# Attention with a threshold and two mixing layers: the order of SyncE's transfers in an attention pair, and filler matmuls at the start

## The chip, the core and the metric

One core of a Trainium2 chip runs the whole kernel. Its engines are TensorE (PE in the rows, with PEld for its weight loads), VectorE (DVE), ScalarE (ACT), GpSimd (POOL) and SyncE (SP), whose instructions here only issue transfers to the core's DMA engines. The metric is the time of one execution in microseconds (us), the median of several.

## The reference

Eight batches of eight heads, 576 positions, head size 64. Attention keeps only the scores within tau of their row's maximum:

```python
scores = scale * np.matmul(q, k.transpose(0, 1, 3, 2))          # (8, 8, 576, 576)
thresh = np.max(scores, axis=-1, keepdims=True) - tau
scores = np.where(scores >= thresh, scores, -1000000000.0)
attn = np.exp(scores - np.max(scores, axis=-1, keepdims=True))
attn = attn / (np.sum(attn, axis=-1, keepdims=True) + 1e-09)
x = np.matmul(attn, v)                                          # then (8, 576, 512)
```

Two mixing layers follow on x. The first mixes each position with the one before it, multiplies by w_k (512 to 1024), squares the positive part, multiplies by w_v, and gates the result with a sigmoid of a product with w_r. The second gates x @ w_val with the sigmoid of a causal convolution over five positions, and multiplies by w_out.

## The kernel before

The attention stage comes first, then the mixing stage, which starts when attention has ended. Attention works on 32 **pairs** of heads; in pair c both heads share the 128 partitions. Its scores are made in nine tiles, scores0 to scores8, of 128 rows by 576 columns each, in three PSUM slots.

Each engine has a written-out order of steps for one turn of the loop, `run(it, c)`; a step marked `-` in a plan belongs to the pair before. In turn c:

- **TensorE** follows `PE_PLAN`: probs5 of the pair before, then scores1, k0, kq0 (transposes of the next pair's k and of the remainders), scores0, pv0 of the pair before (the product with v), q0, and so on. `scores1` is the first product that needs the stacked q and k of its pair.
- **VectorE** takes a tile's maximum (L651), later its mask with the row sum (L656), and once a pair, between mask8 of the pair before and mask1, the reciprocal of all row sums (L662).
- **ScalarE** takes the exponential (L586) and copies every transposed tile out of PSUM (L568, L572).
- **GpSimd** has one queue of work in each turn. With `with_w` (24 turns, c - 3 counts them) it begins with one block of the mixing weights, which it splits into a high and a low part:

```python
def run(it, c, with_w=False):
    if with_w:
        split_w(it, c - 3)          # waits for w_stage (L414, L416)
    if c > 0:
        sums(it, c - 1)             # row_sum + 1e-9 (L421); the reciprocal waits for it
    if c < PAIRS - 1:
        split_k(it, c + 1, c)       # k_hi, k_lo of the next pair (L405, L408)
        if c == 0:
            wait(q_stacked[0], 32)
        split_q(it, c + 1, c)       # q_hi, q_lo of the next pair (L394, L396)
    if c > 0:
        normalize(it, c - 1)        # x_out = x_raw * recip_rows (L429, L432)
```

- **SyncE** issues, in program order and waiting where a transfer's source isn't ready: q and k of pair c + 2 (`load_q`, `load_k`, six transfers), the reciprocals of pair c - 1 to DRAM (`send_recip`, two), the halves of k_lo and k_hi of pair c + 1 that change partitions (`stack_k`, four), the same for q (`stack_q`, L257 and L258, waits for q_lo), the reciprocals of pair c - 1 back as rows spread over partitions (`fetch_rows`, L320, two transfers), v of pair c + 1 (`load_v`, three), a block of weights into the single buffer `w_stage` (`load_w`, L300, one) and x of pair c - 1 to DRAM (`store_x`, L305, waits for x_out).

At the very start TensorE has nothing to do while the first q and k arrive, are transposed and split. `keep_busy(n)` issues n products of the identity with itself into a score slot, whose result nobody reads; each shows as two matmuls in the trace. `FIRST_PREPARE` is the steps k0, kq0, q0; it runs for pair 0 and then for pair 1, ahead of the first scores.

Of the kernel before, what the change touches and what calls it, by code (L numbers as in the profile page):

```python
# [21 lines left out]
def steps(text):  # L22

    return [(w.rstrip("-")[:-1], int(w.rstrip("-")[-1]), w.endswith("-")) for w in text.split()]
# [16 lines left out]
FIRST_PREPARE = steps("k0 kq0 q0")  # L41
# [40 lines left out]
def attention(nc, q, k, v, tau, small_loads, x_first, weights, x_scratch, recip_scratch, w_hi, w_lo):  # L82

    B, H, S, D = q.shape
    PAIRS = B * H // 2
# [9 lines left out]
    with ExitStack() as ctx:  # L95
# [78 lines left out]
        def count(it, c, per_pair, local):  # L174
            return it * (2 * per_pair) + (c * per_pair + local)
# [33 lines left out]
        def turns(it, n):  # L209
            return it * (2 * PER_PAIR) + n  # L210
# [33 lines left out]
        def load_q(eng, it, c):  # L244
            load_qk(eng, 0, "q", it, c, q_loaded)
# [7 lines left out]
        def stack_q(eng, it, c):  # L253

            par = c % 2
            eng.wait_ge(q_steps, count(it, c, 3, 3))
            eng.dma_start(q_all[REM:P, par, 0:QW].bitcast(F32), q_lo[0:REM, :].bitcast(F32)).then_inc(q_stacked[c % 2], 16)  # L257
            eng.dma_start(q_all[0:REM, par, H1:].bitcast(F32), q_lo[REM:P, :].bitcast(F32)).then_inc(q_stacked[c % 2], 16)  # L258
# [10 lines left out]
        with nc.Block() as block:  # L269

            @block.sync
            def _(sp):
# [18 lines left out]
                def load_w(it, c, w, at):  # L291


                    n = c - 2
                    sp.wait_ge(w_split, count(it, n, 2, 2))
                    if w.shape[1] == UNIT:
                        rows, col = it * (2 * P) + (n - at) * P, 0
                    else:
                        rows, col = it * P - at // 2 * P, n * UNIT
                    sp.dma_start(w_stage[:], w[bass.ds(rows, P), col:col + UNIT]).then_inc(w_loaded, 16)  # L300
# [14 lines left out]
                def fetch_rows(it, c):  # L315

                    rows = recip_scratch[c % 2]
                    sp.wait_ge(recip_stored, count(it, c, 32, 32))
                    for h in range(2):
                        sp.dma_start(recip_rows[D * h:D * (h + 1), :],  # L320
                                     rows[h].partition_broadcast(D)).then_inc(rows_loaded, 16)

                def run(it, c, *weight):
                    if c <= PAIRS - 3:

                        sp.wait_ge(aux_full, turns(it, prepared(c - 1)))
                        load_q(sp, it, c + 2)
                        load_k(sp, it, c + 2)
                    if c > 0:
                        send_recip(it, c - 1)  # L330
                    if c < PAIRS - 1:
                        stack_k(it, c + 1)
                        stack_q(sp, it, c + 1)
                    if c > 0:
                        fetch_rows(it, c - 1)
                    if c < PAIRS - 1:
                        if c > 0:
                            sp.wait_ge(aux_full, turns(it, number_of(c - 1, "pv", 1) + 1))
                        load_v(sp, it, c + 1)
                    if weight:  # L340
                        load_w(it, c, *weight)
                    if c > 0:
                        store_x(it, c - 1)

# [117 lines left out]
            def _(pe):  # L462
# [89 lines left out]
                def keep_busy(n):  # L552


                    for _ in range(n):
                        nc.tensor.matmul(score_ps[2][:, 0, 0:P], ident[:], ident[:], start=True, stop=True)
# [1 line left out]
                keep_busy(9)  # L558
                run(FIRST_PREPARE, 0, -1)
                keep_busy(3)  # L560
                run(FIRST_PREPARE, 0, 0)
                keep_busy(3)
                walk(run, pe, PE_PLAN)

            @block.scalar
# [652 lines left out]
```

## Time and profile before

| | |
|---|---|
| median of 3 runs | 1316.13 us (1315.88 to 1316.9) |
| profiled execution | 1318.56 us, of which the span of its instructions is 1316.7 us |
| PE busy | 1282.7 us, 97% of the span |
| DVE busy | 886.7 us, 67% |
| ACT busy | 842.7 us, 64% |
| POOL busy | 334.5 us, 25% |
| mean share of the clock granted to TensorE | 0.99 |

The times of the runs are of whole executions; the trace covers the span of one of them. A busy share is a mean over the attention stage (roughly the first 585 us) and the mixing stage, which have different limits. PE's busy time counts the whole passage of overlapping matmuls through the array, so a busy PE isn't necessarily one without room.

### The profile page before, as it was taken

To read this page: it belongs to the slowest core of one execution; us is meant where nothing else is said; L and a number is where in the kernel's file an instruction comes from. 1 tells how busy PE (TensorE), PEld (TensorE's weight loads), DVE (VectorE), ACT (ScalarE), POOL (GpSimd) and SP (SyncE) were. 2 spreads that over 40 slices of the span, in tenths; PEclk is the share of its full clock that TensorE was granted. 3 is DMA by queue.
4 is the path that set the end of the run, shared out by engine and by line. 5 is a ranking of instruction groups with operands and counts; after the bars stand their busy time and mean duration, and the time that the engine had idled before them with its cause. 6 is when DMAs were issued, how large, how long until landed. Compare 5 with 4: busy or idle time off the path is not lost.

```text
span 1316.7 us, 29536 instructions
## 1 busy us (share of the span) xinstructions
PE 1282.7 (97%) x9358; PEld 1134.5 (86%) x9358; DVE 886.7 (67%) x1969; ACT 842.7 (64%) x2023; POOL 334.5 (25%) x385
## 2 busy tenths in 40 slices
PE   7999999999999999979999999999999999999998
PEld 6778777777777777759999999999989999999997
DVE  4777777777777777758666665657655766566644
ACT  4888888888888888866544453445445544544432
POOL 2466555666665554512000000000000000000000
PEclk7999999999999999999999999999999999999999
DMA  6455656665656655421001101110110011001000
GB/s 148 109 148 151 158 152 158 155 155 151 149 148 161 161 146 144 120 80 53 9 27 36 35 9 37 35 35 1 35 44 18 19 35 35 17 27 35 17 9 33
DMA packets 137821, 105.19 MB, mean 80 GB/s; under 512 B 92416, under 2 KB 109056, under 8 KB 137728
## 3 DMA queue, kind: packets, MB, share of 16 engines
q1 hardware_dynamic: 136224, 103.41, 29.4%
q8 instruction: 49, 0.80, 0.3%
q10 hardware_dynamic: 1504, 0.62, 0.2%
q14 instruction: 44, 0.36, 0.1%
HBM read 54.56 MB, written 19.02 MB: 56 GB/s over the span
## 4 chain that ended last, share of the span: by engine, by line
PE 54%; ACT 0%; DVE 0%; issue 0%; DVEq 0%
PE kv_ps L894 16%; PE kv_ps L975 15%; PE vr_ps L894 15%; PE y_ps L959 8%; ACT mixed L1007 0%; DVE x L1146 0%; ACT xm_hi L1015 0%; ACT y L1024 0%; DVE mixed L1087 0%; DVE square L1104 0%; DVE g_lo L1119 0%; DVE x_lo L1151 0%; DVE xm_lo L1093 0%; DVE gated L1114 0%; ACT g_hi L1055 0%
## 5 line engine op out<-in xcount | busy, mean ns | idle before, releaser
L656 DVE SCALAR_TENSOR_TENSOR probs<-score_ps,threshold,probs 128x576 f32<-128x576 f32 x288 | 227.9, 808 | 44.3 <-ACT probs L586 44.2
L651 DVE TENSOR_REDUCE neg_max<-score_ps 128x1 f32<-128x576 f32 x288 | 211.8, 753 | 53.9 <-PE score_ps L505 53.9
L586 ACT ACTIVATE probs<-score_ps,neg_max 128x576 f32<-128x576 f32 x288 | 213.5, 741 | 0.0
L505 PE MATMUL score_ps<-k_lo,q_all 128*128 128x288 f32 x640 | 195.7, 335 | 8.1 <-DVE probs L656 6.7
L568 ACT ACTIVATE probsT<-aux_ps 128x512 f32<-128x512 f32 x288 | 165.1, 600 | 38.2 <-PE aux_ps L466 33.9
L466 PE MATMUL aux_ps<-ident,probs 128*128 128x128 f32 x1280 | 185.0, 276 | 0.1
L505 PE MATMUL score_ps<-k_hi,q_all 128*128 128x288 f32 x640 | 173.8, 299 | 0.0
L466 PEld LDWEIGHTS aux_ps<-ident,probs 128*128 128x128 f32 x1280 | 150.7, 141 | 17.1 <-ACT probsT L568 15.2
L894 PE MATMUL kv_ps<-xm_hi,w_lo 128*128 128x288 f32 x512 | 152.0, 297 | 10.3 <-DVE xm_lo L1093 7.3
L894 PE MATMUL kv_ps<-xm_hi,w_hi 128*128 128x288 f32 x512 | 152.1, 297 | 0.0
L894 PE MATMUL kv_ps<-xm_lo,w_hi 128*128 128x288 f32 x512 | 151.9, 297 | 0.0
L975 PE MATMUL kv_ps<-kk_hi,w_hi 128*128 128x288 f32 x512 | 151.1, 295 | 0.0
L975 PE MATMUL kv_ps<-kk_lo,w_hi 128*128 128x288 f32 x512 | 150.9, 295 | 0.0
L975 PE MATMUL kv_ps<-kk_hi,w_lo 128*128 128x288 f32 x512 | 150.2, 293 | 0.0
L1159 DVE SCALAR_TENSOR_TENSOR gate<-x,taps,gate 128x288 f32<-128x288 f32 x256 | 132.1, 516 | 18.8 <-ACT gate L1044 15.3
L546 PE MATMUL aux_ps<-probsT,v_nat 128*64 128x320 f32 (+1 forms) x1024 | 138.3, 412 | 2.9 <-ACT probsT L568 1.2
L884 POOL MEMSET x_in<- 128x4 f32 x7 | 0.7, 106 | 539.2 <-DVE mixed L1087 539.2
L505 PEld LDWEIGHTS score_ps<-k_lo,q_all 128*128 128x128 f32 x640 | 119.2, 192 | 15.4 <-DVE probs L656 13.2
L505 PEld LDWEIGHTS score_ps<-k_hi,q_all 128*128 128x128 f32 x640 | 119.9, 193 | 0.0
L546 PEld LDWEIGHTS aux_ps<-probsT,v_nat 128*64 128x64 f32 x1024 | 68.8, 136 | 52.7 <-issue 6.4
L1044 ACT ACTIVATE gate<-x,taps 128x288 f32<-128x288 f32 x64 | 34.1, 533 | 115.4 <-DVE x L1146 115.4
L894 PEld LDWEIGHTS kv_ps<-xm_hi,w_lo 128*128 128x128 f32 x512 | 97.2, 190 | 11.5 <-DVE xm_lo L1093 7.9
(93 smaller groups left out, 2953.4 us busy)
## 6 DMA issues: line engine op xcount, KB each, us to landing
q_all<-q_lo SPq DMA_DIRECT2D x62, 160.0 KB, 2.6
recip_rows<-recip_scratch SPq DMA_DIRECT2D x64, 144.0 KB, 3.2
x_scratch<-x_out SPq DMA_DIRECT2D x32, 288.0 KB, 2.1
out<-y SPq DMA_DIRECT2D x36, 256.0 KB, 2.0
v_nat<-in_v SPq DMA_DIRECT2D x32, 256.0 KB, 2.9
qk_nat<-in_q SPq DMA_DIRECT2D x63, 128.0 KB, 2.6
qk_nat<-in_k SPq DMA_DIRECT2D x63, 128.0 KB, 2.6
k_hi<-k_hi SPq DMA_DIRECT2D x32, 160.0 KB, 2.6
```

The source lines that it names most:

```text
L466: return nc.tensor.transpose(out, in_, ident[:])
L505: last = nc.tensor.matmul(ps[:, half, 0:HALF], query(h, i, par), kk[:, par, at:at + HALF], start=(n == 0), stop=(n == len(terms) - 1))
L546: last = nc.tensor.matmul(bank[D * h:D * (h + 1), 0:cols.stop - cols.start], v_nat[rows, cc % 2, h * FULL + t if t < FULL else MIX, :], m, ...
L568: return nc.scalar.activation(out, in_, ACT.Copy)
L586: nc.scalar.activation(tile_halves(i), scored(i), ACT.Exp, bias=neg_max[:, i:i + 1], scale=1.0).then_inc(exp_done, 1)
L651: nc.vector.tensor_reduce(neg_max[:, i:i + 1], scored(i), mybir.AxisListType.XY, ALU.max, negate=True).then_inc(max_ready, 1)
L656: nc.vector.scalar_tensor_tensor(tile_halves(i), scored(i), threshold[:, i:i + 1], tile_halves(i), ALU.is_ge, ALU.mult, accum_out=row_sum[ ...
L894: last = nc.tensor.matmul(ps, w, m, start=(n == 0), stop=(n == 3 * len(terms) - 1))
L959: last = nc.tensor.matmul(y_ps[i % 2][:], g[:, ch, col:col + P], w[:, ch, :], start=(n == 0), stop=(n == 3 * C - 1))
L975: last = nc.tensor.matmul(kv_ps[u][:, 0:HT], w, m[:, j, :], start=(n == 0), stop=(n == 3 * CF - 1))
L1044: nc.scalar.activation(gate[:, i, :], x2[:, i, 0:HT], ACT.Copy, scale=taps[:, 0, i:i + 1]).then_inc(conv_begun, 1)
L1159: nc.vector.scalar_tensor_tensor(gate[:, u, :], x2[:, u, t:t + HT], taps[:, t, u:u + 1], gate[:, u, :], ALU.mult, ALU.add).then_inc(conv_s ...
```

## The change

SyncE's order in a turn is changed in two places. `fetch_rows` now stands ahead of `stack_q`, and `load_w` ahead of `load_v` and of the wait that guards `load_v`. The transfers themselves, their sizes and what they wait for are the same. On TensorE the fillers at the start change: fifteen now stand between kq0 and q0 of pair 1, and seven where three stood ahead of the first scores.

```diff
                     if c < PAIRS - 1:
                         stack_k(it, c + 1)
-                        stack_q(sp, it, c + 1)
                     if c > 0:
                         fetch_rows(it, c - 1)
+                    if c < PAIRS - 1:
+                        stack_q(sp, it, c + 1)
+                    if weight:
+                        load_w(it, c, *weight)
                     if c < PAIRS - 1:
                         if c > 0:
                             sp.wait_ge(aux_full, turns(it, number_of(c - 1, "pv", 1) + 1))
                         load_v(sp, it, c + 1)
-                    if weight:
-                        load_w(it, c, *weight)
                     if c > 0:
                         store_x(it, c - 1)
...
                 keep_busy(3)
-                run(FIRST_PREPARE, 0, 0)
-                keep_busy(3)
+                run(FIRST_PREPARE[:-1], 0, 0)
+                keep_busy(15)
+                run(FIRST_PREPARE[-1:], 0, 0)
+                keep_busy(7)
                 walk(run, pe, PE_PLAN)
```

This is SyncE's queue in a turn of the loop with weights, before the change; the names are destination and source of a transfer, and the rows without DMA compute addresses and semaphore values.

```order
L279 DMA k_hi<-k_hi 64x640
L256 ISA
L257 DMA q_all<-q_lo 64x640
L258 DMA q_all<-q_lo 64x640
L318 ISA
L320 DMA recip_rows<-recip_scratch 64x576 x2
L338 REGISTER_ALU
L219 ISA
L219 DMA v_nat<-in_v 128x2x256
...
L300 ISA
L300 DMA w_stage<-in_moe_w_k 128x512
```

And this is the same place after the change.

```order
L279 DMA k_hi<-k_hi 64x640
L318 ISA
L320 DMA recip_rows<-recip_scratch 64x576 x2
L256 ISA
L257 DMA q_all<-q_lo 64x640
L258 DMA q_all<-q_lo 64x640
L295 REGISTER_ALU
L300 ISA
L300 DMA w_stage<-in_moe_w_k 128x512
L341 REGISTER_ALU
L219 ISA
L219 DMA v_nat<-in_v 128x2x256
```

The two row fetches have moved ahead of the two q copies, and the weight block ahead of the three transfers of v. Turns without weights show the same move without the L300 rows.

TensorE's queue at the start, before the change, from the fillers between the preparations of pair 0 and pair 1 (`ident,qk_nat` x4 is k0 the first time and q0 the second, `ident,rem_nat` is kq0):

```order
L556 MATMUL score_ps<-ident 128x128 x3
L466 MATMUL aux_ps<-ident,qk_nat 128x128 x4
L466 MATMUL aux_ps<-ident,rem_nat 128x128
L466 MATMUL aux_ps<-ident,qk_nat 128x128 x4
L556 MATMUL score_ps<-ident 128x128 x3
L505 MATMUL score_ps<-k_lo,q_all 128x288
```

After the change:

```order
L557 MATMUL score_ps<-ident 128x128 x3
L467 MATMUL aux_ps<-ident,qk_nat 128x128 x4
L467 MATMUL aux_ps<-ident,rem_nat 128x128
L557 MATMUL score_ps<-ident 128x128 x15
L467 MATMUL aux_ps<-ident,qk_nat 128x128 x4
L557 MATMUL score_ps<-ident 128x128 x7
L506 MATMUL score_ps<-k_lo,q_all 128x288
```

Fifteen fillers now precede q0 of pair 1, and the run of fillers ahead of the first score product has grown from three to seven.

## Rows read from the trace of the kernel before

**Rows 1.** Windows, with and without weights: us, busy us (instructions) by engine.

```profile
53.60:476.10 422.50, 417.16 (x3225) 322.86 (x3222) 320.16 (x673) 371.42 (x866) 259.31 (x289) 1.00 0.60 154
...
492.40:561.30 68.90, 68.55 (x535) 53.15 (x535) 53.69 (x112) 60.89 (x143) 35.70 (x41) 1.00 0.51 133
```

**Rows 2.** Waits, 53.7 to 476 us: total us, times, longest.

```profile
POOL x_out L429 <- DMA recip_rows<-recip_scratch: 103.4, 19, 7.3
DVE recip L662 <- POOL row_sum L421: 36.6, 24, 2.4
...
PEld score_ps L505 <- DVE probs L656: 8.3, 19, 1.1
```

**Rows 3.** Waits, 476 to 561 us.

```profile
POOL row_sum L421 <- DVE probs L656: 8.8, 4, 2.5
```

**Rows 4.** Timeline of DVE: start, us, instruction, idle before and releaser.

```profile
53.64 0.21 DVE L662 RECIPROCAL recip<-row_sum 128x9 f32<-128x9 f32 x1 [0.44 <-POOL row_sum L421]
...
492.51 0.21 DVE L662 RECIPROCAL recip<-row_sum 128x9 f32<-128x9 f32 x1 [0.44 <-POOL row_sum L421]
...
561.38 0.21 DVE L662 RECIPROCAL recip<-row_sum 128x9 f32<-128x9 f32 x1 [0.45 <-POOL row_sum L421]
```

**Rows 5.** Timeline of POOL, one period of a pair with weights.

```profile
265.82 0.25 POOL L421 TENSOR_SCALAR row_sum<-row_sum 128x9 f32<-128x9 f32 x1
...
271.83 1.55 POOL L396 TENSOR_TENSOR q_lo<-q_raw,q_all 128x640 fp32r<-128x640 f32 x1
...
278.61 1.30 POOL L429 TENSOR_TENSOR x_out<-x_raw,recip_rows 128x512 f32<-128x512 f32 x1 [5.24 <-DMA recip_rows<-recip_scratch]
...
281.10 0.61 POOL L414 CAST w_hi<-w_stage 128x512 f32 x1 [0.92 <-DMA w_stage<-in_moe_w_v]
...
283.31 0.25 POOL L421 TENSOR_SCALAR row_sum<-row_sum 128x9 f32<-128x9 f32 x1
```

**Rows 6.** Timeline of SP's queue, the same period: start, us of issuing.

```profile
272.42 0.60 SPq L279 DMA_DIRECT2D k_hi<-k_hi  x1
...
273.40 0.46 SPq L257 DMA_DIRECT2D q_all<-q_lo  x1
...
274.62 1.15 SPq L320 DMA_DIRECT2D recip_rows<-recip_scratch  x2
...
278.13 0.36 SPq L300 DMA_DIRECT2D w_stage<-in_moe_w_v  x1
```

**Rows 7.** Landing times: the second q copy (L258).

```profile
DMA to landing us min/median/max: 2.6/2.7/4.0
```

**Rows 8.** Landing times: the row fetches (L320).

```profile
DMA to landing us min/median/max: 2.8/3.2/3.9
```

**Rows 9.** Timeline of SP's queue, a pair without weights.

```profile
516.63 0.60 SPq L279 DMA_DIRECT2D k_hi<-k_hi  x1
```

**Rows 10.** Timeline of PE, scores1 of the pair after it.

```profile
522.70 0.40 PE L505 MATMUL score_ps<-k_lo,q_all 128*128 128x288 f32 x1
```

**Rows 11.** Timeline of PE at the start: start, us, instruction, idle before.

```profile
7.96 0.83 PE L556 MATMUL score_ps<-ident 128*128 128x128 f32 x6
...
12.53 0.66 PE L466 MATMUL aux_ps<-ident,qk_nat 128*128 128x128 f32 x4 [3.19 <-ACT k_raw L568]
...
15.11 0.61 PE L505 MATMUL score_ps<-k_lo,q_all 128*128 128x288 f32 x1 [0.99 <-DMA q_all<-q_lo]
```

**Rows 12.** Windows around the clock's changes; PEclk stands after POOL.

```profile
13.40:13.50 0.10, 0.10 (x4) 0.10 (x3) 0.00 (x0) 0.10 (x1) 0.10 (x1) 0.72 1.01 149
...
30.50:31.00 0.50, 0.50 (x6) 0.50 (x5) 0.43 (x1) 0.37 (x2) 0.00 (x0) 0.99 0.00 0
```

**Rows 13.** Timeline of DVE at the start: the first maximum.

```profile
16.48 0.76 DVE L651 TENSOR_REDUCE neg_max<-score_ps 128x1 f32<-128x576 f32 x1 [5.34 <-PE score_ps L505]
```

**Rows 14.** Timeline, a score group and its maximum at the full clock.

```profile
270.16 0.38 PE L505 MATMUL score_ps<-k_lo,q_all 128*128 128x288 f32 x1
...
270.97 0.76 DVE L651 TENSOR_REDUCE neg_max<-score_ps 128x1 f32<-128x576 f32 x1 [0.49 <-PE score_ps L505]
```

## The prediction

> **What bounds the kernel now.** The change acts on the attention stage, so I read that stage alone, first as windows. Over the pairs with weights TensorE counts as busy for 417.16 of 422.50 us, over those without for 68.55 of 68.90; DVE and ACT have room in both [rows 1]. That looks like a stage bound by TensorE whatever SyncE does. But busy time counts overlapping passages, so I went on to how long a pair takes. The reciprocal comes once a pair. From 53.64 to 492.51 us there are 25 periods (the 24 with weights and the one that follows them), 438.87 us, 17.55 each; from 492.51 to 561.38 four without weights, 68.87 us, 17.22 each [rows 4]. The same products therefore take 0.33 us longer per pair when GpSimd also has a weight block to split, and this difference is what the change can reach.
>
> The waits name the place. With weights the reciprocal waits for GpSimd's row_sum 24 times, 36.6 us together, or 1.5 us each, where the hand-over alone costs 0.44 when GpSimd is in time [rows 2, 4]. TensorE's score weights wait for a mask 19 times, 8.3 us [rows 2]; that is the late reciprocal passed on, for mask1 stands behind it. Without weights it is the other way round: row_sum waits 2.2 us for VectorE (8.8 us in four) [rows 3].
>
> Why is GpSimd late? I followed one period back. row_sum starts at 265.82; the work behind it, the splits of k and q, ends with q_lo, which starts at 271.83 and takes 1.55, so 273.38 [rows 5]. At 273.40 SyncE issues the q copies, at 274.62 the row fetches, then v, and at 278.13 the weight block [rows 6]. GpSimd gets the rows at 278.61 and the weights at 281.10, and the next row_sum comes at 283.31 [rows 5]. This is a closed loop: 7.56 (row_sum to the end of q_lo) + 0.02 (the queue answers) + 1.22 (q copies) + 3.51 (row fetches and v) + 2.97 (the weights' flight) + 2.21 (split) = 17.49 us, the whole distance from 265.82 to 283.31. With weights the bound is thus a ring over GpSimd, SyncE's queue and one transfer, slightly longer than the 17.22 that the rest of the stage needs.
>
> **The change, part by part.** *Row fetches ahead of the q copies.* The fourth k copy is issued from 272.42 to 273.02 [rows 6]. Before, the queue then stood until q_lo was ready, at 273.40; now the fetches go at about 273.05, 1.57 us sooner, and rows that came at 278.61 come near 277.0. x_out and its small second part fill the time from 278.61 to about 280.2 now (1.6 us, its first part 1.30), so GpSimd would be free at 278.6. *Weights ahead of v.* Fetches to 274.2, q copies to 275.4, weight block issued at about 275.5 instead of 278.13. With the same flight of 2.97 it lands at 278.5, as GpSimd becomes free. Then 2.21 us of splitting puts row_sum at 280.8 instead of 283.31, 2.5 us sooner. It was 1.5 - 0.44 = 1.1 us late on average, so it will be in time with about 1.4 to spare, even in the worst turn (2.4 - 0.44 = 2.0 us late [rows 2]). The ring shrinks to about 15.0 us and stops binding. Next comes whatever gives the pairs without weights their 17.22. I take that value: (438.87 - 25 x 17.22) = 438.87 - 430.5 = **8.4 us gained**. Bounds: 0, if weights slow the stage in another way, and 9 or so, since nothing in rows 4 shows a pair faster than 17.2 for a reason that would stay.
>
> *v later.* Its three transfers slip by roughly 0.6 us in a turn with weights (one weight issue of 0.36 and its addresses), and are used a pair later; I cost this at nothing, covered by nearly a whole period. Without that cover it would be 0.6 us a pair.
>
> *The q copies later.* This is the price of the exchange. In a pair without weights the fourth k copy ends at 516.63 + 0.60 = 517.23 [rows 9]. Two fetches (1.15) and the first q copy (about 0.55) now stand ahead of the second q copy, with the gaps it is issued at about 519.2. With its median flight of 2.7 [rows 7] it lands at 521.9, and scores1 of the next pair begins at 522.70 [rows 10]: 0.8 us of room. Flight may grow behind 288 KB of fetches. The fetches, the nearest transfers that now fly behind others, take 3.2 [rows 8]; at 3.2 there is still 0.3. I cost it at nothing, with the bounds 0 and 0.5 us a pair (flight 4.0, the longest seen [rows 7]).
>
> The Trainium skill speaks to this ("DMA: Bandwidth & Descriptors", section "Queues, rings and completion order"): on each DMA engine the descriptors of one issuing queue are consumed in ring order. By that rule the q copies can't overtake the fetches, and every byte of these stands before them; the sum by the rule alone has the room of 0.8 us less whatever the fetches' data take, which brings the slower rival below nearer. The row of the second q copy, 2.7 us behind four k copies and a first q copy, shows that standing behind others cost little so far.
>
> *The fillers.* TensorE stood idle for 3.19 us ahead of q0 of pair 1, and the granted clock then fell to half inside the window at 13.40 and came back only inside 30.50 to 31.00 [rows 11, 12]. Six filler matmuls took 0.83 us at the full clock [rows 11], at a spacing of about 0.12 once the passage of the last is taken off. Fifteen fillers are 30 matmuls, 3.6 us, from about 9.2 to 12.8: they fill the idle time and push q0 from 12.53 to about 12.8. q0 isn't urgent, GpSimd comes to it after the k splits. Seven are 14 matmuls, 1.7 us, so TensorE is free at about 15.0, and the scores start at 15.11 as before, when the q copy has landed [rows 11]. If the fillers ran longer, 0.14 each, the scores would start 0.8 us late: that is the loss side. The gain: with the half clock the first maximum came 16.48 - 15.11 = 1.37 us after the first score product [rows 11, 13], at the full clock this takes 270.97 - 270.16 = 0.81 [rows 14]. That is 0.56 us at the first tile. In the idle-ridden stretch that follows VectorE sets the pace, and the clock may well fall again; if it stayed full to 30 us, I'd add two more such first tiles (1.1) and half of roughly 3 us of score and transpose work back to back: 2.8 in all. Between -0.8 and 2.8 I take **0.9**, near the term that I can name.
>
> **Sum.** 8.4 + 0.9 = 9.3 us. The profiled execution took 1318.56 us, 1316.7 of span and 1.86 around it; it would become 1309.3. It stands 2.43 above the median of the runs, so for the median 1316.13 - 9.3 = **1306.8 us**. One term without a sign: as the mixing stage begins, the clock's return depends on when the work falls, and may move the end by about 1 us either way (my estimate, from the 0.56 us that one tile at half clock costs).
>
> **The rivals.**
>
> *The q copies come too late.* Mechanism: scores1 waits for q_stacked at the head of every pair, some 30 pairs. It decides when the flight of the second q copy exceeds 522.70 - 519.2 = 3.5 us. At 4.0 each of 30 pairs loses 0.5 us, 15 us against 9.3 gained: 1321.8, slower. For it: the transfers are issued nearly as fast as they are served, and 4.0 has occurred. Against: 2.7 is the median and even the fetches take 3.2. Slower than before takes over 3.9 us; 5 in 100 for that, 5 more for a loss that eats only half the gain.
>
> *The weighted pairs keep part of their extra.* The ring is broken, but other waits, such as ScalarE's or the DMA engines' greater share with weights (0.60 against 0.51 [rows 1]), hold the period at about 17.4. Half of 8.4 is left, 1311.0. 14 in 100.
>
> *The change doesn't do it.* TensorE counts as busy 99% of the time both with and without weights [rows 1]; if that were its true load, earlier rows and weights would only give GpSimd idle time, and only the start would move: 1315.2. Against it stands the ring's sum, which equals the measured period. 7 in 100.
>
> *The clock holds through the first 30 us.* 8.4 + 2.8: 1304.9. 15 in 100. My forecast, 1306.8 within 2 us, keeps 54.
>
> **How the numbers follow.** The point is the forecast. The range of 8 in 10 reaches down past the case of the held clock with a share of the 1 us at the seam, to 1302.5, and up to cover the case of half the gain, 1312.5; outside are the unchanged case and the slow end of the late copies above, and something below. About 0.2%, 2.6 us, is what a measurement of this kernel tells from no change. Faster by more than that needs a time below 1313.5: 54 + 15 + 14 and half of the late copies, together 0.87; the same 0.08; slower 0.05.
>
> **What would show it right or wrong.** In the changed profile the reciprocal's idle time should be 0.44 in nearly all turns, row_sum should be released by VectorE's probs instead of following w_lo, and the reciprocal's period should be about 17.2 from the first turn to the last. The rows should reach GpSimd some 1.5 us sooner in a turn. Wrong would be a wait of PE's scores1 for the DMA q_all from q_lo, once a pair: then the exchange has made a new head of the ring. At the start PE's idle time ahead of q0 should be gone, the clock full past 13.40, and the first maximum at about 15.9 instead of 16.48.

## The result and the profile after

| | before | after |
|---|---|---|
| median | 1316.01 us (20 runs, 1313.73 to 1319.45 and one of 2775.76) | 1318.4 us (20 runs, 1316.31 to 1322.9) |
| ratio, 95% interval | | 1.0019 (1.0011 to 1.0027) |
| profiled execution | 1318.56 us, span 1316.7 | 1316.92 us, span 1315.1 |

The change makes the kernel 0.19% slower, 2.4 us by the medians, where I had forecast 9.3 us of gain. The one execution of 2775.76 us isn't part of the ratio. The two profiled executions stand the other way round: that of before is 2.5 us above its median, that of after 1.5 us below. A difference of 1.6 us between two profiles therefore doesn't carry the verdict. But the profiles show which stretch gained and which lost. From the head of the changed kernel's page, its span and the busy time of each engine:

```profile
span 1315.1 us, 29612 instructions
...
PE 1282.8 (98%) x9396; PEld 1136.1 (86%) x9396; DVE 891.0 (68%) x1969; ACT 839.9 (64%) x2023; POOL 334.5 (25%) x385
```

Busy times are nearly those of before. DVE has 4 us more with the same number of instructions, a first hint that some of them took longer; ACT has 3 us less. The timeline of DVE shows the reciprocals that answer to [rows 4], now with the last of the 32 as well:

```profile
53.56 0.21 DVE L665 RECIPROCAL recip<-row_sum 128x9 f32<-128x9 f32 x1 [0.45 <-POOL row_sum L422]
...
487.15 0.22 DVE L665 RECIPROCAL recip<-row_sum 128x9 f32<-128x9 f32 x1 [0.45 <-POOL row_sum L422]
...
556.59 0.21 DVE L665 RECIPROCAL recip<-row_sum 128x9 f32<-128x9 f32 x1 [0.45 <-POOL row_sum L422]
...
573.00 0.22 DVE L665 RECIPROCAL recip<-row_sum 128x9 f32<-128x9 f32 x1 [0.44 <-POOL row_sum L422]
```

and the last of the kernel before:

```profile
577.75 0.21 DVE L662 RECIPROCAL recip<-row_sum 128x9 f32<-128x9 f32 x1 [0.43 <-POOL row_sum L421]
```

The reciprocal waits 0.45 us, the bare hand-over, in every pair. From 53.56 to 487.15 there are 25 periods of 17.34 us where there were 17.55. From 487.15 to 556.59 there are four without weights, of 17.36, where there were 17.22. So the pairs with weights gained 0.21 us of the 0.33 that I expected, and those without lost 0.14 each. The first turn, from the first reciprocal (35.26 us) to the second, takes 18.30 us instead of 17.23: it gives back the 1.15 us that the start had won. The last reciprocal comes at 573.00 instead of 577.75 us, and yet the span is only 1.6 us shorter: from that row to the end it takes 742.1 us instead of 739.0. Something after the attention stage lost 3.1 us.

The timeline of POOL for one period with weights, to set against [rows 5]:

```profile
267.75 1.55 POOL L397 TENSOR_TENSOR q_lo<-q_raw,q_all 128x640 fp32r<-128x640 f32 x1
273.53 1.30 POOL L430 TENSOR_TENSOR x_out<-x_raw,recip_rows 128x512 f32<-128x512 f32 x1 [4.23 <-DMA recip_rows<-recip_scratch]
...
275.83 0.61 POOL L415 CAST w_hi<-w_stage 128x512 f32 x1 [0.73 <-DMA w_stage<-in_moe_w_v]
...
278.93 0.25 POOL L422 TENSOR_SCALAR row_sum<-row_sum 128x9 f32<-128x9 f32 x1 [0.98 <-DVE probs L659]
```

q_lo ends at 269.30. The rows come 4.23 us after that instead of 5.23, the weights 6.53 instead of 7.72, and the next row_sum is now released by VectorE, 0.98 us after GpSimd was ready for it. The old ring is open, as forecast. SP's queue around it, in the order of the change (start, us of issuing), to set against [rows 6]:

```profile
268.94 0.60 SPq L279 DMA_DIRECT2D k_hi<-k_hi  x1
269.66 1.16 SPq L320 DMA_DIRECT2D recip_rows<-recip_scratch  x2
270.94 0.51 SPq L257 DMA_DIRECT2D q_all<-q_lo  x1
271.50 0.60 SPq L258 DMA_DIRECT2D q_all<-q_lo  x1
272.39 0.34 SPq L300 DMA_DIRECT2D w_stage<-in_moe_w_v  x1
```

The second q copy is now issued at 271.50, 2.56 us after the issue of the last k copy began; before it went right behind the first q copy of 273.40, that is at 273.9, 1.5 us after the k copy of 272.42. The following lines belong to L258, the second q copy: who waited for it (us, times) and its flight, to set against [rows 7]:

```profile
  PE score_ps L506: 1.7, 6
...
DMA to landing us min/median/max: 2.7/3.5/3.9
```

Its flight has grown from 2.7 to 3.5 us, and PE's scores wait for it six times, 1.7 us together, the first of them at the start.

That count is too low: a wait for several semaphores is put down to only one of them. One pair as an example, the issue of its second q copy and the first weight load of its scores1:

```profile
392.67 0.59 SPq L258 DMA_DIRECT2D q_all<-q_lo  x1
...
396.73 0.19 PEld L506 LDWEIGHTS score_ps<-k_lo,q_all 128*128 128x128 f32 x1 [0.52 <-DVE probs L659]
```

This copy landed 3.85 us after its issue, at 396.52, and the weight load began 0.21 us later, after 0.52 us of idle time that is put down to DVE. I followed all 31 copies that SyncE issues. In the changed kernel TensorE's sequencer (the part that issues its instructions) already stood waiting when the copy landed in 29 of them; the weight load followed at a median of 0.21 us behind the landing, and the engine was idle ahead of it in 26, for 7.0 us together. In the kernel before this median was 1.8 us and the idle time 0.05. The length of a pair follows the landing: 17.21 us with a flight of 3.20 us, 17.29 with 3.55, 17.54 with 3.74, 17.70 with 3.85. So the q copy has become the new head of nearly every pair. At the start, timelines of PE and DVE, to set against [rows 11, 13]:

```profile
8.87 3.51 PE L557 MATMUL score_ps<-ident 128*128 128x128 f32 x30
...
12.65 1.73 PE L557 MATMUL score_ps<-ident 128*128 128x128 f32 x14
14.61 0.40 PE L506 MATMUL score_ps<-k_lo,q_all 128*128 128x288 f32 x1 [0.23 <-DMA q_all<-q_lo]
...
15.44 1.42 DVE L654 TENSOR_REDUCE neg_max<-score_ps 128x1 f32<-128x576 f32 x2 [4.70 <-PE score_ps L506]
```

On TensorE, the 30 filler matmuls took 3.51 us, the 14 took 1.73, close to the 3.6 and 1.7 of the forecast. The scores waited only 0.23 us, and the first maximum came 15.44 − 14.61 = 0.83 us after them.

**The seam between the stages.** This is the place that I had not followed. The mixing stage begins with VectorE and ScalarE preparing the first eight inputs (mixed, xm_hi, xm_lo), while GpSimd splits w_out, which SyncE has just begun to load. Two of VectorE's rows, GpSimd's first row of w_out and the window of 12 us from the first matmul of the stage (at 591.35), in the kernel before (a window's columns are those of [rows 1]: PE, PEld, DVE, ACT and POOL, then PEclk, DMA share and GB/s):

```profile
592.07 0.51 DVE L1087 SCALAR_TENSOR_TENSOR mixed<-x_in,mu,mixed 128x288 f32<-128x288 f32 x1
592.50 0.45 DVE L1093 TENSOR_TENSOR xm_lo<-mixed,xm_hi 128x288 fp32r<-128x288 f32 x1
...
593.10 1.12 POOL L876 CAST w_out_hi<-y 128x512 fp32r<-128x512 f32 x1 [4.00 <-DMA y<-in_moe_w_out]
...
591.35:603.35 12.00, 12.00 (x70) 11.76 (x71) 12.00 (x16) 6.78 (x18) 9.22 (x8) 0.76 0.34 109
```

And the same in the changed kernel, where the first matmul is at 586.74:

```profile
587.08 0.87 DVE L1096 TENSOR_TENSOR xm_lo<-mixed,xm_hi 128x288 fp32r<-128x288 f32 x1
587.87 1.52 DVE L1090 SCALAR_TENSOR_TENSOR mixed<-x_in,mu,mixed 128x288 f32<-128x288 f32 x1
...
586.93 0.71 POOL L879 CAST w_out_hi<-y 128x512 fp32r<-128x512 f32 x1 [2.44 <-DMA y<-in_moe_w_out]
...
586.74:598.74 12.00, 9.95 (x46) 8.91 (x47) 11.72 (x15) 5.96 (x16) 8.34 (x8) 0.61 0.20 57
```

Before, GpSimd's work on w_out's first block began 1.75 us after the first matmul; by then VectorE had got ahead of TensorE, 0.51 us a step. After the change it began 0.19 us after the first matmul, and VectorE's steps took 0.87 and 1.52 us from there on. TensorE starved, as its timeline in the changed kernel shows:

```profile
588.01 0.61 PE L897 MATMUL kv_ps<-xm_hi,w_lo 128*128 128x288 f32 x1 [0.18 <-DVE xm_lo L1096]
...
590.23 0.61 PE L897 MATMUL kv_ps<-xm_hi,w_lo 128*128 128x288 f32 x1 [1.14 <-DVE xm_lo L1096]
...
592.04 0.61 PE L897 MATMUL kv_ps<-xm_hi,w_lo 128*128 128x288 f32 x1 [0.73 <-DVE xm_lo L1096]
```

There are 46 matmuls in the window instead of 70. The granted clock averages 0.61 in it instead of 0.76, so with half clock until it rises TensorE spent 9.4 of the 12 us at 1.2 GHz instead of 5.8. 24 matmuls at the full-clock spacing of 0.13 us are 3.1 us, the loss found above. The three waits for xm_lo are 2.05 us of it; the rest fits the longer time at half clock. No run separates the two, for the waits came with the late clock each time. That two instructions which are independent in the program lengthen each other has a rule in the Trainium skill ("SBUF — State Buffer", section "Who interferes with whom"): a VectorE instruction with two SBUF inputs contends with a GpSimd instruction that reads SBUF (the core's on-chip memory). The rows agree: both kinds of row have two SBUF inputs and grow beside GpSimd's rows only.

### The profile page after: what moved, and what is told of

Read it like the earlier page. It is cut to its first block, busy times and chain, and to the rows that moved or that the text cites. A ratio compares the mean times of both kernels' runs of the same rounds, so it can differ in the third digit from the quotient of the medians.

```text
span 1315.1 us, 29612 instructions
## 1 busy us (share of the span) xinstructions
PE 1282.8 (98%) x9396; PEld 1136.1 (86%) x9396; DVE 891.0 (68%) x1969; ACT 839.9 (64%) x2023; POOL 334.5 (25%) x385
## 4 chain that ended last, share of the span: by engine, by line
PE 54%; DVE 1%; ACT 0%; issue 0%; DVEq 0%
PE kv_ps L897 16%; PE kv_ps L978 15%; PE vr_ps L897 15%; PE y_ps L962 8%; DVE mixed L1090 0%; DVE xm_lo L1096 0%; ACT mixed L1010 0%; DVE x L1149 0%; ACT xm_hi L1018 0%; ACT y L1027 0%; DVE x_lo L1154 0%; DVE square L1107 0%; DVE g_lo L1122 0%; DVE gated L1117 0%; ACT x_hi L1074 0%
## 5 line engine op out<-in xcount | busy, mean ns | idle before, releaser
L897 PEld LDWEIGHTS kv_ps<-xm_hi,w_lo 128*128 128x128 f32 x512 | 97.4, 190 | 14.4 <-DVE xm_lo L1096 11.1
```

The source lines that it names most:

```text
L897: last = nc.tensor.matmul(ps, w, m, start=(n == 0), stop=(n == 3 * len(terms) - 1))
```

## The experiments

All ratios are against the kernel before, timed on the same chip; the three repeats are single executions. For the period with weights I give the mean of the 25 between the second and the 27th reciprocal, as in [rows 4], for the seam the time from the first matmul of the mixing stage to the end. The profile is always one execution.

| kernel | ratio (95%) | period with / without weights | q flight, median | seam to end |
|---|---|---|---|---|
| before | 1 | 17.55 / 17.22 | 2.7 | 725.4 |
| before again | | 17.53 / 17.22 | 2.8 | 725.1 |
| changed | 1.0019 (1.0011–1.0027) | 17.34 / 17.36 | 3.5 | 728.4 |
| changed again | | 17.41 / 17.34 | 3.5 | 728.5 |
| fillers only | 1.0019 (1.0008–1.003) | 17.49 / 17.22 | | 728.3 |
| fillers again | | 17.48 / 17.20 | 2.8 | 729.3 |
| order only | 1.001 (0.9996–1.0025) | 17.43 / 17.24 | 3.5 | 725.5 |
| rows first only | 1.0024 (1.0012–1.0036) | 17.63 / 17.30 | 3.7 | 725.7 |
| weights first only | 0.9949 (0.993–0.9968) | 17.23 / 17.22 | 2.8 | 729.0 |
| before, quiet seam | 0.9992 (0.998–1.0003) | 17.46 / 17.22 | | 725.3 |
| changed, quiet seam | 0.9994 (0.9982–1.0005) | 17.52 / 17.37 | 3.7 | 725.2 |
| weights first, quiet seam | 0.9939 (0.9927–0.9951) | 17.21 / 17.21 | | 725.0 |
| fillers, quiet seam | 0.9989 (0.9977–1.0001) | 17.46 / 17.22 | | 725.9 |
| weights, fillers, quiet seam | 0.9939 (0.9926–0.9953) | 17.20 / 17.22 | | 725.2 |
| 38 filler matmuls at the seam | 1.0018 (1.0006–1.0029) | 17.52 / 17.20 | | 728.9 |
| weights, fillers, quiet seam, plus fillers at the seam | 0.9954 (0.994–0.9967) | 17.20 / 17.22 | | 725.5 |

**The change taken apart.** The fillers alone:

```diff
-                run(FIRST_PREPARE, 0, 0)
-                keep_busy(3)
+                run(FIRST_PREPARE[:-1], 0, 0)
+                keep_busy(15)
+                run(FIRST_PREPARE[-1:], 0, 0)
+                keep_busy(7)
```

> Only the fillers of the change, SyncE's order as before. In the changed kernel's profile the first reciprocal came at 35.26 us instead of 36.41. Theory A (the start gains 1.1 us and nothing else depends on it): the ratio is about 0.999, the reciprocal's periods stay near 17.55 with weights. Theory B (the slower executions of the changed kernel come from the fillers, for instance because they change when the mixing stage starts relative to the clock): the ratio is 1.001 or more although the first reciprocal is early.

Measured: 1318.67 us against 1315.63, ratio 1.0019. The first reciprocal, and the first 12 us of the mixing stage:

```profile
35.41 0.22 DVE L664 RECIPROCAL recip<-row_sum 128x9 f32<-128x9 f32 x1 [0.46 <-POOL row_sum L421]
...
588.50:600.50 12.00, 9.73 (x49) 8.91 (x50) 11.78 (x15) 5.92 (x16) 8.63 (x8) 0.65 0.27 64
```

Theory B holds. The start gained 1.0 us (35.41 instead of 36.41), the window at the seam holds 49 matmuls instead of 70, and the fillers lose 2.5 us by the ratio, 3.0 by the medians.

SyncE's order alone (the fillers as before):

```diff
                         stack_k(it, c + 1)
-                        stack_q(sp, it, c + 1)
                     if c > 0:
                         fetch_rows(it, c - 1)
+                    if c < PAIRS - 1:
+                        stack_q(sp, it, c + 1)
+                    if weight:
+                        load_w(it, c, *weight)
...
-                    if weight:
-                        load_w(it, c, *weight)
```

> Only SyncE's new order, the fillers as before. Theory A (the order shortens the attention stage by about 5 us and the seam to the mixing stage gives it back): the reciprocal's periods are near 17.35 all through, the first matmul of the mixing stage comes about 4 us sooner than the 591.35 us of before, and the ratio is nevertheless near 1.00. Theory C (late q copies cost the gain inside the attention stage in most executions): periods of 17.5 or more, with PE waiting for q_all from q_lo in many pairs, ratio 1.002.

Measured: 1317.18 against 1315.63, ratio 1.001, an interval that includes 1; its executions spread from 1312.98 to 1320.44. The period is 17.43, between the two theories, with PE's scores waiting for q copies 7 times, 3.8 us. Followed copy by copy as above, the sequencer stood waiting at the landing in 29 of 31, with 7.7 us of idle time ahead of the weight loads. The seam is as before, 725.5, so theory A's "the seam gives it back" is wrong for the order; it belongs to the fillers.

The two halves of the order. Row fetches first, weights still behind v:

```diff
                         stack_k(it, c + 1)
-                        stack_q(sp, it, c + 1)
                     if c > 0:
                         fetch_rows(it, c - 1)
                     if c < PAIRS - 1:
+                        stack_q(sp, it, c + 1)
```

> Only the row fetches ahead of the q copies, the weight block still behind v. The q copies pay the price, the weights' transfer, the last link of the ring, is issued no sooner (only the waiting between k and q copies goes). Theory C predicts that this half is the harmful one: flight of the second q copy 3.3 us or more, periods near 17.5, ratio 1.001 to 1.004. Theory A: about the same attention stage as before to 2 us better, and a ratio of 0.998 to 1.000.

Measured: 1318.87 us, ratio 1.0024. Reciprocals from DVE's timeline, and the lines of the second q copy:

```profile
54.95 0.22 DVE L662 RECIPROCAL recip<-row_sum 128x9 f32<-128x9 f32 x1 [0.44 <-POOL row_sum L421]
...
495.80 0.22 DVE L662 RECIPROCAL recip<-row_sum 128x9 f32<-128x9 f32 x1 [0.45 <-POOL row_sum L421]
...
  PE score_ps L505: 7.2, 15
...
DMA to landing us min/median/max: 2.7/3.7/5.0
```

The 25 periods take 440.85 us, 17.63 each, though the reciprocal's wait fell (0.95 us on average over these periods instead of 1.51). The flight of the q copy has a median of 3.7 us and a maximum of 5.0, and PE waits for it 15 times, 7.2 us together; copy by copy it is 29 of 31 again, with 12.8 us of idle time. This half is the harmful one, as theory C says.

Weights first, row fetches still behind the q copies:

```diff
                     if c > 0:
                         fetch_rows(it, c - 1)
+                    if weight:
+                        load_w(it, c, *weight)
                     if c < PAIRS - 1:
...
-                    if weight:
-                        load_w(it, c, *weight)
```

> Only the weight block ahead of v, the row fetches still behind the q copies. By the ring the weights land 2.2 us sooner, so the rows bound GpSimd (rows at 278.6, row_sum at about 282.4 instead of 283.3 in the period that the prediction followed): most of the lateness goes and the q copies are as early as before. Theory C: this is the half that gains, periods near 17.25, ratio 0.993 to 0.996. Theory A (the seam gives back what attention gains): periods near 17.25 too, but a ratio of 0.998 or more.

Measured: 1309.68 us, ratio 0.9949, 6 us faster. From DVE's timeline and the lines of the second q copy:

```profile
53.95 0.22 DVE L662 RECIPROCAL recip<-row_sum 128x9 f32<-128x9 f32 x1 [0.44 <-POOL row_sum L421]
...
484.58 0.22 DVE L662 RECIPROCAL recip<-row_sum 128x9 f32<-128x9 f32 x1 [0.44 <-POOL row_sum L421]
...
DMA to landing us min/median/max: 2.7/2.8/4.1
```

430.63 us for 25 periods, 17.23 each: 8.2 us less than in the profile of before, nearly the whole forecast of 8.4, with the q copies flying 2.8 us as before. In no pair did TensorE's sequencer wait for one. That execution itself took 1314.49, the slowest of its six, and had the slow seam (729.0); I have no profile of a faster one.

**The seam made quiet.** Four kernels (before, changed, weights first, fillers only) got the same edit, which also holds for the later runs that name it. GpSimd waits with w_out until VectorE has prepared all eight inputs, and SyncE loads the next x between the second and third block, which would otherwise be late:

```diff
+                load_wo(0)
+                load_wo(1)
+                sp.wait_ge(mix_done, 2 * C)
+                load_x(0, 1)
+                load_wo(2)
+                load_wo(3)
...
                 nc.gpsimd.memset(x_in[:, :, 0:1], 0.0).then_inc(x_edge, 1)
+                pool.wait_ge(mix_lo_ready, 2 * C)
                 for i in range(C):
```

> The kernel before, with GpSimd's split of w_out held back until all eight first mixes are split (one wait on mix_lo_ready), and SyncE loading the next x between the second and third block of w_out. Seam theory: in the profiles so far VectorE's mixes and splits took 0.86 and 1.52 us instead of 0.45 to 0.52 whenever GpSimd split w_out beside them, and from the first matmul of the mixing stage to the end it took 725.4 us where the first block of w_out came 1.8 us or more after that matmul, and 728.3 to 729.0 where it came within 0.6 us. With the split out of the way every mix should take 0.5 us, the stage should take 723 to 725 us, and the kernel should be 1 to 3 us faster than before. Rival: the difference of 3 us comes from the clock alone (full 5.8 us or 9.3 us after the first matmul); then the ratio stays within 0.001 of 1.

Measured: 1316.2 against 1316.69, ratio 0.9992, no more than the uncertainty. The 1 to 3 us that I expected didn't come: 725.3 us from the first matmul to the end instead of 723 to 725. VectorE's steps stayed at 0.45 to 0.52 us for 5.3 us after the first matmul, where they had for 2.3 before, but TensorE issued 70 matmuls in the window and had a mean clock of 0.76 in either case. The kernel before already had the fast kind of seam. By its ratio this run would fit the rival (the clock alone) too; the run of the fillers below goes on from here.

> The changed kernel with the same quiet seam. Seam theory: what the change lost was given back at the seam, so without the collision it is faster than the kernel before with the quiet seam, by 3 to 5 us. Rival (the loss lies in the attention stage or at the start, in executions slower than the profiled one): it stays 2 to 3 us behind the kernel before with the quiet seam, as the changed kernel stays behind the kernel before.

Measured: 1316.05 us, ratio 0.9994. Against the kernel before with the same seam it is level, neither 3 to 5 us faster nor 2 to 3 slower. The seam explains the whole loss against before, but the gain in the attention stage was missing too: its profile has periods of 17.52 and 17.37 us, and PE's scores wait for q copies 15 times, 5.1 us, with a flight of 3.7. Copy by copy it is 29 of 31, with 11.3 us of idle time; a flight of 3.09 us stands beside a pair of 17.21 us, 3.77 beside 17.51, 4.30 beside 18.14.

> Only the weight block ahead of v, with the quiet seam. The attention stage gains 6 to 8 us as before with this half (ratio 0.9949), the seam another 1 to 3: ratio 0.992 to 0.994. If the seam's kind does not matter for the time, 0.995.

Measured: 1309.5 us, ratio 0.9939. DVE's timeline, two reciprocals and two steps at the seam:

```profile
53.62 0.21 DVE L662 RECIPROCAL recip<-row_sum 128x9 f32<-128x9 f32 x1 [0.44 <-POOL row_sum L421]
...
483.77 0.21 DVE L662 RECIPROCAL recip<-row_sum 128x9 f32<-128x9 f32 x1 [0.44 <-POOL row_sum L421]
...
584.01 0.45 DVE L1101 TENSOR_TENSOR xm_lo<-mixed,xm_hi 128x288 fp32r<-128x288 f32 x1
584.38 0.51 DVE L1095 SCALAR_TENSOR_TENSOR mixed<-x_in,mu,mixed 128x288 f32<-128x288 f32 x1
```

17.21 us a pair, and 0.45 to 0.51 us a step with GpSimd out of the way. The ratio lies at the upper end of what I expected. The order's useful half is worth 7.2 us beside the kernel before, 6.7 us beside the same kernel with the quiet seam.

> Only the fillers, with the quiet seam. If the fillers alone lost 3 us (ratio 1.0019) because they turn the seam into the slow kind, this is as fast as the kernel before with the quiet seam or 1 us faster. If they lose in the attention stage, it is 3 us slower than that.

Measured: 1315.72 us, ratio 0.9989. With the quiet seam the fillers no longer lose anything (725.9 us from the first matmul on, 70 matmuls in the window, mean clock 0.76), so the late clock and the loss at the seam both need GpSimd's work beside VectorE's. If the fillers win, it is under 1 us and not told apart from nothing.

**Repeats and the sum of the parts.**

> The kernel before once more, for a second profile. If the kind of seam belongs to the kernel, the first block of w_out comes 1.7 us or more after the first matmul of the mixing stage again, and from that matmul to the end it takes 725 to 726 us. If it changes from execution to execution, either kind can show.

Measured: 1317.47 us; w_out's first block 1.81 us after the first matmul, 725.1 us to the end: the fast kind again.

> The changed kernel once more. If the seam's kind belongs to the kernel: w_out's first block within 0.6 us of the first matmul, 728 to 729 us from there to the end. For the attention stage: median flight of the second q copy 3.5 us or more and row_sum in time, and a period between 17.3 and 17.55 us that depends on how often that flight is over 3.6 us.

Measured: 1318.12 us; w_out's first block 0.33 us after it, 728.5 to the end. The q flight is 3.5 again, with nine waits of PE's scores in the view and 29 of 31 copy by copy, and the period 17.41.

> Only the fillers, once more. If the seam's kind belongs to the kernel: w_out's first block within 0.6 us of the first matmul, 728 to 729 us to the end, while the first reciprocal comes at about 35.4 us.

Measured: 1318.36 us; 0.32 us after it, 729.3 to the end. The kind of seam comes back with the kernel in all three repeats. The first reciprocal came at 34.14 us, not at 35.4 as I had expected, 2 us sooner than without the fillers; in this execution the half clock lasted from 22 to 25 us, where the changed kernel had it from 19 to 29.5.

> The weight block ahead of v, the row fetches behind the q copies as before, the quiet seam, and the fillers of the change. If the three effects are separate they add: the weights 0.9939 with the quiet seam, and the fillers another 0.5 to 1 us, so a ratio of 0.993 to 0.9935 and periods of 17.2 us. If the fillers only shift when idle time falls, it is the same as without them.

Measured: 1308.4 us (1307.67 to 1308.77), ratio 0.9939. Weights first, rows as before, quiet seam and the change's fillers: the lowest median of all kernels here, 8 us under before. The ratio misses the 0.993 to 0.9935 that I expected of a sum. It is the same as without the fillers (1309.5, ratio 0.9939), so no gain of theirs is shown.

**What moves w_out.** The fillers at TensorE's start neither issue nor use the transfer of w_out, and yet it lands sooner with them. In the kernel before a packet of another queue stands beside the transfer. The DMA queues in the 1.2 us after w_out's first issue at 589.00 (packets, MB, share of the 16 engines):

```profile
q1 hardware_dynamic: 17, 0.03, 11.9%
q8 instruction: 1, 0.02, 7.2%
```

Such a q8 packet, of the queue that the profile calls instruction, was there in five profiles (before twice, order only, rows only, before with the quiet seam), and in these w_out's first block landed 3.9 to 4.5 us after its issue. It was missing in all the others, and in these the block landed after 2.5 to 2.9 us. So I took the 38 additional filler matmuls to where TensorE is idle anyway, behind its last attention product:

```diff
                 walk(run, pe, PE_PLAN)
+                keep_busy(19)
```

> The kernel before with the same number of additional filler matmuls as in the change, 38 (19 fillers), but at the end of TensorE's attention program, where it is idle for 7.3 us, instead of at the start. Code theory: the amount of TensorE code ahead of the mixing stage decides where its instruction fetch falls, so w_out's first block lands 2.5 us after its issue as in the kernels with the fillers, no q8 packet stands behind that issue, and VectorE's early mixes take 0.86 and 1.52 us. Place theory (the fillers at the start act through the earlier clock or the earlier first pair): w_out's first block lands 4.1 us after its issue as in the kernel before. The fillers also keep TensorE busy for 4.5 us of the idle time, so the clock may fall later; that is worth up to 3 us by itself and is why the landing and not the time decides.

Measured: 1320.15 against 1316.09, ratio 1.0018. A row of DVE, one of POOL and the window from the first matmul on:

```profile
592.08 1.52 DVE L1094 TENSOR_TENSOR xm_lo<-mixed,xm_hi 128x288 fp32r<-128x288 f32 x1
...
591.17 0.67 POOL L877 CAST w_out_hi<-y 128x512 fp32r<-128x512 f32 x1 [2.85 <-DMA y<-in_moe_w_out]
...
590.57:602.57 12.00, 9.63 (x41) 8.60 (x42) 11.72 (x15) 5.97 (x16) 8.51 (x8) 0.57 0.23 62
```

The run shows what the code theory forecast: w_out's first block lands 2.9 us after its issue instead of 4.0, no q8 packet stands behind that issue, VectorE's step takes 1.52 us and the window holds 41 matmuls. The clock was still full at the first matmul here, fell 0.2 us later and stayed at half for 10 us. So 38 more matmuls go with the quick landing in either place. The amount of code isn't the whole rule: in weights first, with as many instructions as before, the packet was missing too, in both its profiles without fillers, and with the usual seam (one profile) it had the slow kind. What decides when the packet comes stays open.

> The kernel with the weight block ahead of v, the quiet seam and the fillers at the start (ratio 0.9939), with 29 more fillers (58 matmuls, 6.8 us at the full clock) in TensorE's idle time before the mixing stage. In the profiles the clock falls there and comes back 4 to 11 us after the first matmul of the stage, and a matmul of 288 columns is started every 0.24 us instead of 0.13. If the clock stays full: 2 to 3 us faster, ratio 0.9915 to 0.9925, and from the first matmul to the end 722 to 723 us instead of 725.2. If it falls anyway: the same ratio as without, 0.994.

```diff
                 walk(run, pe, PE_PLAN)
+                keep_busy(29)
```

Measured: 1310.66 us, ratio 0.9954. That is no faster than without them (0.9939) and by the two ratios 2 us slower, though the intervals overlap. The fillers kept the clock full at the first matmul, but it fell 2.0 us later and was back at 5.4. They ended at 580.8 us, and GpSimd's and VectorE's first instructions of the mixing stage, which had come 2.5 us after the last store's issue, now came 4.5 us after it: the stage starts when TensorE is done too. From the first matmul to the end it took 725.5 us, not the expected 722 to 723.

## Why the prediction was wrong

**What bounds the kernel now: right.** The ring over GpSimd, SyncE's queue and the weights' transfer set the period. With the ring opened (weights first) the period fell to 17.20 to 17.23 us in all four kernels that have that half alone, the next bound of 17.22. The size was too large. I took 8.4 us from a profile that stood 2.4 us above the median, and subtracted them from the median. The profile of before with the quiet seam, an execution of 1316.31 us at its median, has periods of 17.46, and 25 x (17.46 - 17.22) = 6.0 us. The medians agree with that: weights first measured 6.0 to 7.2 us of gain.

***Row fetches ahead of the q copies* and *weights ahead of v*: right in direction, but only the second was needed.** In the changed kernel row_sum came in time in every pair. "2.5 us sooner" was more than needed, and the 1.1 us required were to be had from the weights alone.

***The q copies later*, "I cost it at nothing": the first step that failed.** I had put the second q copy 0.8 us ahead of its need with the old flight of 2.7, and 0.3 with 3.2, the fetches' flight. The 4.0 of [rows 7] that I took as the longest was no measure of either: it is the first copy, which ScalarE issues at 11.1 us, and none of SyncE's 31 took more than 2.84. Behind the fetches it flew 3.5 to 3.7 us in the median, up to 4.3 in the changed kernel with the quiet seam and 5.0 with the rows alone. The time of issue was right (1.96 us after the end of the last k copy, 271.50 − 269.54, as I had put it), and so was the 3.5 us which the first rival named as its point of decision; the flight was the term that I had wrong. So the rival came true in part. The sign that I had named for it, a wait of scores1 once a pair, is in the traces: TensorE's sequencer waited for the landing of 29 of 31 copies in all five profiles with the fetches first, and in at most 2 of 31 in the eleven others. The idle time ahead of the weight loads was 7.0 to 12.8 us against at most 0.06. Periods in the profiles of the changed kernel were 17.34 to 17.52 us instead of 17.22, which over 25 periods is 3 to 7.6 us. With the quiet seam on both sides no gain at all was left: 0.9994 against 0.9992. The Trainium skill's rule on ring order that I weighed ("DMA: Bandwidth & Descriptors", section "Queues, rings and completion order") pointed the right way. The row that I set against it, 2.7 us behind k copies, was no measure, for the flight of the same copy rose by 0.8 us as soon as the fetches went ahead.

***The fillers*, 0.9 us: right at the start, wrong in the whole.** The first reciprocal came at 34.14 to 35.66 us in the kernels with these fillers, at 36.17 to 36.66 in those without. The half clock came at about 19 us instead of 13.4, so of my cases it was the one where it falls again. In the changed kernel the gain didn't last beyond the first turn, where the late q copy took it back. What I had left out is that 38 more matmuls in the program go with another kind of seam. "One term without a sign ... 1 us either way" was the only place where I touched it, and I sized it from the clock alone; the collision between GpSimd and VectorE there cost 3 us, in each profile of a kernel with these 38 matmuls and no quiet seam. That is the second step that failed, and it decided the sign: the fillers alone measure 1.0019, as the whole change does.

**The sum.** The two first profiles add up exactly. First reciprocal −1.15 us, first turn +1.07, 25 periods −5.28, four pairs without weights +0.57, from there to the mixing stage +0.18, the stage itself +3.0: −1.6, the difference of the spans.

For the medians the sum is looser, with terms of single executions: start −1, ring −6.0, late q copies +3.1 to +7.6 in the 25 periods, +0.3 to +1.1 in the first turn and about +0.5 in the pairs without weights, seam +3. That is between −0.1 and +5.2 us, and the measured +2.4 lies inside. Three places thus separate the forecast of −9.3 from it: 2.4 us in the ring's size, 4 to 9 in the q copies, 3 at the seam.

**The order of the rivals.** I gave the late copies 10 in 100 and let them act alone; that the total came out near the case of no change is the sum of a gain and two losses, and not what that case describes. I had named their place and point correctly, and then called 0.3 to 0.8 us of room safe for 30 pairs, with no measured flight in that position.

## What to carry to other kernels

Before moving a transfer behind others in one queue, compare its room with its flight in the new position, not the old one: here 0.8 us of room was used up by 288 KB of fetches. When a change has two halves, build each, since here the half that moved one small issue gave 6 to 7 us and the other took most of them back. And when the profiled execution stands above the median, don't subtract a gain read from its profile from the median. Look at the seams between stages, too, after every change of a program: 38 matmuls in a place that had time for them went with a loss of 3 us almost six hundred microseconds later, and one wait that orders the two engines there made the time independent of it.

## What the runs showed of the hardware

- VectorE's steps of 288 columns with two SBUF inputs, 0.45 to 0.52 us alone, took 0.86 and 1.52 us beside GpSimd's cast and subtraction of w_out. In the window of 12 us TensorE issued 39 to 49 matmuls instead of 68 to 70, and its clock, which in all but one of these profiles had fallen to 1.2 GHz in the idle time before, averaged 0.53 to 0.65 of full instead of 0.74 to 0.76.
- A single packet of the instruction queue (0.02 MB) next to a transfer of 256 KB goes with a later landing: 3.9 to 4.5 us in the five profiles that have it, 2.5 to 2.9 in the eleven without. That the packet is the cause wasn't tried by itself. It was missing in all kernels with 38 or more matmuls added, and in those with the weights first.
- The same q copy took 2.7 to 2.8 us behind k copies and 3.5 to 3.7 behind two row fetches of 144 KB (medians). TensorE's first weight load that needs it began 0.2 us after its landing in 29 of 31 cases.
